# A fused attention, MLP and routed-expert kernel: attention written out tile by tile, logits computed in column groups, and the turned constants moved across the wait for the scatter

## The reference

```python
# attention with decay, B=2, H=8, S=768, D=48, step by step over t
cur   = einsum('bhd,bhe->bhde', u * kt, vt)
y[t]  = einsum('bhd,bhde->bhe', rt, state + cur)
state = w * state + einsum('bhd,bhe->bhde', kt, vt)
# x = y as 1536 rows of 384
h = x @ w_in                                   # 384 x 2048
x = (max(h, 0) + alpha * min(h, 0)) @ w_out    # 2048 x 384
# routed experts: E=8, F=1024, capacity 384
logits = x @ w_gate                            # 384 x 8
e = argmax(logits); gate = softmax(logits)[e]
# rows go to their expert in order; then
out = gate * (max(rows @ w1[e], 0) @ w2[e])
```

## Time and profile before

| quantity | value |
|---|---|
| median of 3 runs | 457.8 us |
| lowest, highest | 457.57, 458.06 us |
| profiled execution, device time | 459.43 us |
| profiled execution, span | 457.7 us |
| PE busy | 428.1 us (94%) |
| DVE / ACT / POOL busy | 255.0 / 198.1 / 180.0 us |

### The profile page before, as it was taken

One profiled execution on the slowest core, in us unless ns is written; L12 is line 12 of the kernel. 1 busy time (PEld: TensorE's weight loads), 2 busy tenths in 40 slices (PEclk: granted clock), 3 DMA queues, 4 the chain that ended last, 5 costly groups with the idle time before them and its releaser, 6 DMA issues.

```text
span 457.7 us, 9164 instructions
## 1 busy us (share of the span) xinstructions
PE 428.1 (94%) x3133; PEld 416.5 (91%) x3133; DVE 255.0 (56%) x548; ACT 198.1 (43%) x450; POOL 180.0 (39%) x196
## 2 busy tenths in 40 slices
PE   2799999999999999999999996989999999998891
PEld 2688889999999999999999996989999999998891
DVE  4667886766425334253345665264478584658620
ACT  0689864342311113111233333144567674558640
POOL 4879945554312623235355670530110210013112
PEclk9799999999999999999999998899999999999997
DMA  6876414545980100001003351493676876563000
GB/s 252 313 244 211 136 38 157 161 129 175 364 288 0 53 0 0 0 9 43 0 1 94 103 165 36 156 367 97 205 225 192 258 208 185 168 205 90 9 19 7
DMA packets 34219, 61.38 MB, mean 134 GB/s; under 512 B 4654, under 2 KB 27486, under 8 KB 34176
## 3 DMA queue, kind: packets, MB, share of 16 engines
q1 hardware_dynamic: 30720, 55.23, 37.8%
q0 software_dynamic: 3456, 5.59, 3.9%
HBM read 47.53 MB, written 14.79 MB: 136 GB/s over the span
## 4 chain that ended last, share of the span: by engine, by line
PE 82%; DVE 6%; ACT 5%; issue 4%; POOL 1%; DMA 0%; ACTq 0%; DVEq 0%; POOLq 0%
PE bank L1129 19%; PE bank L1144 18%; PE bank L1245 17%; PE bank L1274 14%; ACT scores L604 3%; PE bank L1284 2%; PE bank L1099 2%; PE bank L1056 2%; PE bank L1161 2%; PE bank L1232 1%; ACT w_high L587 1%; PE bank L1090 1%; DVE neg L870 1%; PE bank L1043 1%; DVE act_full L876 1%
## 5 line engine op out<-in xcount | busy, mean ns | idle before, releaser
L500 POOL TENSOR_TENSOR g_low<-act_full,g_high 128x384 fp32r<-128x384 f32 x63 | 63.7, 1010 | 116.8 <-ACT g_high L636 116.8
L636 ACT ACTIVATE g_high<-act_full 128x384 fp32r<-128x384 f32 x64 | 33.6, 526 | 152.8 <-DVE act_full L876 142.9
L1129 PE MATMUL bank<-x_split,w_high 128*128 (+1 forms) x384 | 98.2, 336 | 0.0
L870 DVE TENSOR_SCALAR neg<-bank,alpha_sb 128x384 f32<-128x384 f32 x64 | 39.2, 613 | 73.4 <-PE bank L1129 73.4
L556 POOL DMA_INDIRECT out<-y_out,token x24 | 24.7, 1030 | 123.4 <-ACT y_out L723 119.8
L1129 PEld LDWEIGHTS bank<-x_split,w_high 128*128 128x128 f32 x384 | 69.0, 188 | 0.2 <-issue 0.2
L1144 PE MATMUL bank<-w_high,g_high 128*128 128x384 f32 x189 | 64.7, 342 | 1.2 <-POOL g_low L500 1.2
L1129 PE MATMUL bank<-x_split,w_low 128*128 (+1 forms) x192 | 64.4, 335 | 0.0
L1144 PE MATMUL bank<-w_low,g_high 128*128 128x384 f32 x189 | 63.8, 338 | 0.0
L1144 PE MATMUL bank<-w_high,g_low 128*128 128x384 f32 x189 | 63.7, 337 | 0.0
L1245 PE MATMUL bank<-xe_high,w_high 128*128 128x256 f32 (+1 forms) x192 | 58.0, 302 | 1.8 <-DVE xe_low L981 1.8
(11 more groups left out here) (121 smaller groups left out, 810.1 us busy)
## 6 DMA issues: line engine op xcount, KB each, us to landing
w_raw<-chunks SPq DMA_DIRECT2D x96, 192.0 KB, 2.8
w_raw<-chunks SPq DMA_DIRECT2D x32, 384.0 KB, 3.2
rk_in<-att_rk SPq DMA_DIRECT2D x12, 704.0 KB, 4.5
routed_rows<-fill SPq DMA_DIRECT2D x1, 5211.0 KB, 17.9
xe<-routed_rows SPq DMA_DIRECT2D x7, 579.0 KB
v_in<-att_v SPq DMA_DIRECT2D x12, 200.0 KB, 4.7
out<-fill SPq DMA_DIRECT2D x1, 2304.0 KB, 23.2
x_split<-x_split POOLq DMA_DIRECT2D x24, 48.0 KB, 2.5
```

The source lines that it names most:

```text
L500: pool.tensor_tensor(gl[:, f % 4, :], act_full[:, f % 2, :], gh[:, f % 4, :].bitcast(f32), ALU.subtract).then_inc(s_gl, 1)
L636: act.activation(gh[:, f % 4, :], act_full[:, f % 2, :], ACT.Copy).then_inc(s_gh, 1)
L870: dve.tensor_scalar(neg[:, f % 2, :], h, 0.0, alpha_sb[:, f:f + 1], ALU.min, ALU.mult)\
L1129: last = mm(bank[f % 4][:, 0:G], a[:, f, w], x[:, kc, bass.ds(g * G, G)], start=kc == 0 and i == 0, stop=kc == KC - 1 and i == 2)
```

## The change

1. The attention loop is written out: the 12 tiles are Python iterations, with constant semaphore values, no branches and no register arithmetic (`reuse` waits only where something is to be waited for). In this form DVE's low half of tile 5 comes behind the mask of tile 6, which was the other way round across the loop's end.
2. `rk_in` and `r_hat` have four buffers instead of three.
3. The start: PE turns constants 22 times (`START_WARM`) as soon as `ident` is there. The last doubling of the powers is cut in two, the r half first. The turned powers go to bank 6, so that `k_turn(0)` no longer waits for `pw_u`. DVE makes the first `rw` itself and copies the second `kn`. POOL's order becomes k_hat, rw, r_hat. ACT casts `after_b` first.
4. ACT's four early weight splits move from tiles 2 to 5 to tiles 6 to 9. The six DMAs that move pieces of the first group go from POOL to SP.
5. The logits: `wg_sb` (8 columns) is now the stationary operand and the rows are the moving one (128 columns). The three row tiles write to the partitions from 0, 32 and 64. DVE copies the 72 rows to SBUF and PE turns them back. `choose` moves from f = 4 to f = 5, `gate_exp` from 5 to 6, `positions` behind `down(4)`, `x2t_copy` ahead of `g_high(3)`.
6. `keep_warm` before the experts: 6 and eight times 3 ahead of the wait for the scatter, 24 behind it.

```diff
-    WARM = 6
+    WARM = 3
+    START_WARM = 22
+    RK = 4
+    RH = 4
...
             pe.wait_ge(s_const, CONSTS)
-            pe.wait_ge(s_pow, POWERS)
+            keep_warm(START_WARM)
+            pe.wait_ge(s_pow, R_POWERS)
             for a in range(PAIRS):
-                last = pe.transpose(misc[:, a * P:(a + 1) * P], pw[:, 0, a, 1:P + 1], ident[:, :])
+                last = pe.transpose(bank[6][:, a * P:(a + 1) * P], pw[:, 0, a, 1:P + 1], ident[:, :])
             last.then_inc(s_pwx, 1)
...
+            pool.wait_ge(s_khat, 1)
+            pool.wait_ge(s_rb, 1)
+            r_hats(0)
+            pool.wait_ge(s_rw, 1)
+            for t in range(1, T):
+                k_hats(t)
+                rws(t)
+                r_hats(t)
...
             dve.wait_ge(s_const, CONSTS)
-            dve.tensor_copy(after_b[:, :], after[:, :]).then_inc(s_cast, 1)
-            bonus_sums(0, 0)
-            bonus_sums(0, 1)
-            with dve.Fori(0, B) as b:
-                for c in range(CT):
-                    mask(b, c)
-                    if c < CT - 1:
-                        new_state(b, c)
-                    if c:
-                        x_low(b, c - 1)
-                    ahead(dve, b, c, 2, bonus_sums)
...
+            for t in range(T):
+                mask(t)
+                if t % CT < CT - 1:
+                    new_state(t)
+                if t:
+                    x_low(t - 1)
+                if t + 2 < T:
+                    bonus_sums(t + 2)
...
             def logits(q):
-                for i in range(GT):
-                    pe.wait_ge(s_x2t, q * GT + i + 1)
-                    for kc in range(KC):
-                        last = mm(LG[:, i, :], x2t[:, i, kc * P:(kc + 1) * P], wg_sb[:, kc, :],
-                                  start=kc == 0, stop=kc == KC - 1)
-                last.then_inc(s_lg, 1)
+
+                pe.wait_ge(s_x2t, q * GT + GT)
+                for kc in range(KC):
+                    for i in range(GT):
+                        last = mm(LGT[i * COL:i * COL + E, :], wg_sb[:, kc, :], x2t[:, i, kc * P:(kc + 1) * P],
+                                  start=kc == 0, stop=kc == KC - 1, skip_group_check=True)
+                last.then_inc(s_lgt, 1)
+
+            def turn_logits(q):
+
+                pe.wait_ge(s_lgc, q + 1)
+                pe.transpose(misc[:, 0:ROWS], x2t[0:ROWS, 0, 0:P], ident[0:ROWS, 0:ROWS]).then_inc(s_lg, 1)
...
             pe.wait_ge(s_g, FFN_STEPS)
-            keep_warm(WARM)
+            keep_warm(2 * WARM)
...
                 keep_warm(WARM)
 
             pe.wait_ge(s_scat, 16 * T)
-            keep_warm(3 * WARM)
+            keep_warm(8 * WARM)
```

More of the change, by code:

```diff
@@ L114, in attention_moe_kernel @@
     state = spare.take("state", [P, 2, PAIRS, HALF], f32)
+    kn = spare.take("kn", [P, 2, PAIRS * P], f32)
+    rw = spare.take("rw", [P, 2, DM], f32)
+    ruk = spare.take("ruk", [P, 2, DM], f32)
     v_in = spare.take("v_in", [P, CT, DM + PAD], f32)
@@ L159, in sem @@
             return ctx.enter_context(nc.semaphore(name))
-        s_rk = [sem(f"rk_loaded{i}") for i in range(3)]
+        s_rk = [sem(f"rk_loaded{i}") for i in range(RK)]
         s_v = [sem(f"v_loaded{i}") for i in range(CT)]
@@ L600, in diagonals @@
+            def diagonals(t):
                 act.wait_ge(s_bon, t + 1)
-                act.wait_ge(s_y, t - 1 + C_Y)
+                reuse(act, s_y, t - 1)
                 for h in range(H):
-                    last = act.activation(scores[:, c % 2, h % 2, h // 2, :], ident[:, :], ACT.Copy,
-                                          scale=diag[:, c % 2, h:h + 1])
+                    last = act.activation(scores[:, t % 2, h % 2, h // 2, :], ident[:, :], ACT.Copy,
+                                          scale=diag[:, t % 2, h:h + 1])
@@ L615, in _ @@
             act.wait_ge(s_const, CONSTS)
-            kn_copy(0, 0)
-            kn_copy(0, 1)
-            diagonals(0, 0)
-            with act.Fori(0, B) as b:
-                for c in range(CT):
-                    if c:
-                        x_high(b, c - 1)
-                    ahead(act, b, c, 2, kn_copy)
-                    ahead(act, b, c, 1, diagonals)
-                    if c >= CT - EARLY:
-                        with act.If(b < 1):
-                            split_high(c - CT + EARLY)
-                x_high(b, CT - 1)
+            act.activation(after_b[:, :], after[:, :], ACT.Copy).then_inc(s_cast, 1)
@@ L658, in group @@
                         x2_copy(g - 1)
-                    if split != "mlp" and f == 4:
+                    if split != "mlp" and f == 3:
                         x2t_copy(g - 1)
@@ L663, in group @@
                         split_high(f + EARLY)
-                    if split != "mlp" and f == 5:
+                    if split != "mlp" and f == 6:
                         gate_exp(g - 1)
@@ L756, in _ @@
         def _(dve):
[L757 removed]
+            for s, n in ((s_mgl, C_MGL),):
                 dve.sem_inc(s, n)
@@ L930, in group @@
                     if split != "mlp" and f == 4:
+                        logits_copy(g - 1)
+                    if split != "mlp" and f == 5:
                         choose(g - 1)
@@ L1099, in stage2 @@
                         last = mm(yb[h2 * HALF:(h2 + 1) * HALF, a * P:(a + 1) * P], v_in[:, c, h * D:h * D + HALF],
-                                  scores[:, c % 2, h2, a, :], start=c == 0 and a == 0, stop=True,
+                                  scores[:, t % 2, h2, a, :], start=c == 0 and a == 0, stop=True,
                                   skip_group_check=True)
                 last.then_inc(s_y, 1)
+            k_turn(0)
+            scored(0)
+            update(0)
+            k_turn(1)
             pe.wait_ge(s_pwu, 1)
-            k_turn(0, 0)
-            scored(0, 0)
-            update(0, 0)
-            k_turn(0, 1)
-            with pe.Fori(0, B) as b:
-                for c in range(CT):
-                    ahead(pe, b, c, 2, k_turn)
-                    ahead(pe, b, c, 1, scored)
-                    stage2(b, c)
-                    ahead(pe, b, c, 1, update)
+            for t in range(T):
+                if t + 2 < T:
+                    k_turn(t + 2)
+                if t + 1 < T:
+                    scored(t + 1)
+                stage2(t)
+                if t + 1 < T and (t + 1) % CT < CT - 1:
+                    update(t + 1)
             def up(g, f):
@@ L1197, in group @@
                     down(g, f)
-                if q is not None:
-                    positions(q)
+                    if q is not None and f == 0:
+                        turn_logits(q)
                 for f in range(5, NF):
@@ L1202, in group @@
                     down(g, f - LAG)
+                    if q is not None and f == 6:
+                        positions(q)
             pe.wait_ge(s_par, 32)
             pe.wait_ge(s_cast, 1)
-            pe.wait_ge(s_masked, T + C_MASK)
+            pe.wait_ge(s_masked, T)
             group(0, None)
@@ L1279, in expert_down @@
                     last.then_inc(s_yd[i], 1)
-            def keep_warm(n):
-                for _ in range(n):
-                    pe.transpose(bank[0][:, 0:P], ident[:, :], ident[:, :])
             pe.wait_ge(s_g, FFN_STEPS)
-            keep_warm(WARM)
+            keep_warm(2 * WARM)
             pe.wait_ge(s_cnti, 1)
```

329 lines of the change are left out of this document (167 added, 162 removed).

## The result

| | median us | lowest to highest, runs | profiled execution: time, span |
|---|---|---|---|
| before | 457.93 | 457.57 to 460.13, 6 | 459.43, 457.7 |
| changed | 454.5 | 453.29 to 456.75, 6 | 453.51, 451.8 |

The ratio is 0.9915 (95% interval 0.9891 to 0.9939). The changed kernel is faster by about 3.4 us in the medians and by 5.9 in the spans of the two profiled executions. The forecast was 453.7, in a range of 450.6 to 456.4. In a second batch the medians were 459.52 and 454.26, 5.3 us apart.

What follows compares the result with a forecast made beforehand. PE was taken as the bound in later attention, with chains over several engines at the start and last group's routing. Gains 3.4 (attention) + 1.95 (logits) - 1.25 (routing to experts) = 4.1 us: 455.3 profiled, 453.7 median, range 450.6 to 456.4.

Steps and rivals of the forecast that it cites:

- Start of attention: Start relay to tile 1's output: 22.6 us instead of 25.71, one tile in a low clock stretch, 3.1 us gained.
- the best case: Start of attention with the higher clock from 14 us on: tile 1's output at 21.5, 4.2 us earlier.
- the rival of a weak start: Constants do not help, PE's clock stays low until 20 us and more: 2.0 gained instead of 3.1; chance 0.14.
- Tile 5 to tile 6: Attention outputs of tiles 5 and 6: 3.1 us apart instead of 4.66 with the mask first, 1.5 us gained.
- The 0.2 at tile 5: Attention, tile 5: 0.2 us more gained because the weight split is gone from it.
- Splits at the end: ACT's four splits in tiles 6 to 9: last two outputs 3.5 us apart instead of 2.1, 1.4 us lost.
- Logits: Three boundaries: nine products 1.15 us instead of 1.91, turn back 0.11, so 0.65 us gained each, 1.95 in all.
- that rule: Rival for the logits: column groups run beside each other, nine products about 0.4 us, 2.2 us better; chance 0.09.
- Last group and constants: Routing before the experts: 0.35 us lost in the last group's chain, 0.6 gained by rearranging the turned constants.
- the 0.6: Expert 0's first product at 298.55 instead of 299.16: PE turns two row tiles early, then waits for the third.
- The clock at the experts: Expert 0's first products: clock falls after PE's idle time before them, 1.5 us lost; forecast case, chance 0.40.
- holding: Rival at the experts: the clock does not fall, 1.5 us better, 452.2 us; chance 0.32.

Runs made afterwards that it cites:

- old logits: Changed kernel with the logits computed as before (rows stationary, 8 columns moving, choose at f = 4): 460.95 us, ratio 1.0047.
- 40 at the start: Changed kernel with START_WARM 40 in place of 22, 18 more constants turned at PE's head: 455.23 us, ratio 0.9919.
- by row tile: Changed kernel with the nine logit products ordered by row tile instead of by k chunk: 456.8 us, ratio 0.9961.
- the two with early splits: Changed kernel with ACT's four weight splits back in tiles 2 to 5: 453.83 us; the same plus 54 and 18 constants at the routing: 452.12 us.
- old mask: Changed kernel with DVE's low half of tile 5 ahead of the mask of tile 6, as before: 454.08 us, ratio 0.9923.
- 72 constants: Changed kernel with 54 turned constants ahead of the wait for the scatter and 18 behind it, as before: 451.71 us, ratio 0.9856.
- filled pause: Changed kernel with 18 more constants turned in PE's pause behind tile 0's second k_turn: 452.44 us, ratio 0.9858.

## Why the prediction was right, and where it was not

The time was right to 0.8 us, and that was partly luck: three gains were forecast too small, a forecast loss did not occur in the profile, and a loss that no step named took their place. Luck also lies in the translation to medians: in the profiled executions the gain was 5.9 us and not 4.1, in the medians 3.4.

- *Start of attention*: 3.1 us forecast, 3.4 measured. The value chosen (output of tile 1 at 22.6, one tile in a low stretch) was the right case: 22.32. What it called the best case also exists, 21.1 us, in the executions where the clock held behind the same pause. The clock did not stay low to 20 us, so the rival of a weak start is refuted for the changed kernel. Without the start constants it did stay low until about 19 us, and tile 1's output came at 23.07, so they carry 0.8 us of the 3.4.
- *Tile 5 to tile 6*: 1.5 forecast and 1.50 measured. But the reason given, the order of the mask, carries 0.70 of it and alone would bring 0.1 to the end of attention. The forecast took PE for the bound here; behind tile 5 the chain is ACT's, from 40.66 to 59.25 us of the changed kernel, its diagonals above all. The 0.2 at tile 5 came (0.20), though not from the weight splits, since it stays with the splits in their old place.
- *Splits at the end*: 1.4 lost forecast, 0.96 measured and 1.0 won back by undoing it. Mechanism right, size too large by nearly half.
- *Logits*: the term that was mis-sized. I priced nine products at 64 ns a record, 1.15 us; they took 0.77, and a boundary gained 0.88 in place of 0.65 (the two rows, 0.77 and 0.07 for 1.91, would give 1.07; the stretch shows 0.2 less, and why is open). The Trainium skill ("TensorEngine Tiling (Array Packing)", Tiling Modes) has column tiles work in parallel; the trace agrees in kind, since turning the order cost 0.44 us, and not in size, since by that rule I had reckoned 0.4 us. I compared with a product that alternates between column halves and did not overlap; it is another shape, and should not have stood for this one.
- *Last group and constants*: -0.35 forecast, -0.26 measured; 0.6 forecast, 0.83 measured. The reason given for the 0.6 did not hold: PE was to turn two row tiles early and wait for the third. The constants ended 9.5 us behind the count and not 8.5 (24 of them took 5.29 us at the low clock, the rest came in runs between reads of the counts), the third tile landed 3.5 us at most behind its issue and not 4.0, and PE waited 0.2 us for it.
- *The clock at the experts*: a fall of 1.5 us, chance 0.40, against holding, 0.32. In the changed kernel's two profiled executions it held. The step that failed is the overlap ahead of it: I had PE idle for 3.0 of the 4.0 us from 294.5 on; measured is 1.7 of 2.8 us (288.99 to 291.81), with a longest pause of 1.69 us, inside the 1.85 us that had passed without a fall before. The mechanism and its price exist: the fall came in five of the eleven other profiled executions (old logits, 40 at the start, by row tile, and the two with early splits), each time at 1.5 to 1.6 us. The length of the pause does not decide: the clock fell with old logits, where the only pause there was 1.61 us, and held with the old mask, where PE waited 1.50 us for the third tile and then 1.57 us. What decides is open.
- *Not foreseen*: 1.92 us in the experts, late first down products that hang on where PE's code lies; that instruction transfers hold them is argued, not shown. Without it and with the clock as it was, the profiled span would have been 449.9, an estimate.

Measured terms: 4.1 + 2.64 - 0.26 + 0.83 = 7.3 us, less 1.9, plus 0.5 at the end. The forecast's 3.4 + 1.95 - 1.25 = 4.1.

## What to carry to other kernels

Price an edit by its own rows in the trace and not by the difference of two medians: here 18 harmless instructions moved up to 2 us elsewhere, and undoing under 3 us of logits moved the time by 6. In a chain of waits that ends in "issue" behind a branch, look for an instruction transfer about 3 us ahead before blaming the named releaser, and move the code by a few instructions to test it: a transfer just ahead is no proof by itself. Work in narrow column groups should go to the groups in turn.

## What the runs showed of the hardware

- The first down product behind a jump came up to 2.68 us late at experts 1 to 3, and in all 25 such cases it started 2.9 to 3.6 us behind a 16 KB transfer on the instruction queue. The down products themselves took as long with a pause as without (8.40 to 8.43 us from first down to next up).
- Nine products of 8 stationary and 128 moving columns: 0.77 us into three column groups in turn, 1.21 us group by group.
- The same code of PE, with a pause of 2.3 to 2.6 us from 12.6 us on, was followed by a fall of the clock to 0.50 for about 3 us in four executions (the changed kernel's two, old logits, old mask) and by none in four others (72 constants, by row tile, the two with early splits). It costs 1.2 to 1.6 us at tile 1's output. The 22 constants at the start had taken 4.95 to 4.96 us in the first four and 4.31 to 4.73 in the others. With the filled pause they took 4.60 us, and the clock fell even so, before that pause; what decides is not shown.
- A semaphore increment on PE's list took 0.15 us: 32 of them from 0.91 to 5.71 us.
